# A Fourier transform and two MLPs: the feature transform folded into the first weights, the 64-point transform moved into the first block

## The reference

```
X = np.fft.fft(np.fft.fft(x, axis=1), axis=2).real
h = X @ w_in;   g = np.where(h > 0, h, np.exp(np.minimum(h, 0)) - 1);   x = g @ w_out
h = x @ w_in2;  g = np.maximum(h, 0) + alpha * np.minimum(h, 0);         out = g @ w_out2
```

## Time and profile before

| what | us |
|---|---|
| times of three runs | 1038.32, 1039.86, 1041.12 |
| median | 1039.86 |
| span of the profiled execution | 1040.5 |
| TensorE busy | 1018.8 (98% of the span) |
| ScalarE busy | 673.9 (65%) |
| VectorE busy | 652.1 (63%) |
| POOL busy | 112.6 (11%) |

### The profile page before, as it was taken

One profiled execution on the slowest core, in us unless ns is written; L12 is line 12 of the kernel. 1 busy time (PEld: TensorE's weight loads), 2 busy tenths in 40 slices (PEclk: granted clock), 3 DMA queues, 4 the chain that ended last, 5 costly groups with the idle time before them and its releaser, 6 DMA issues.

```text
span 1040.5 us, 13229 instructions
## 1 busy us (share of the span) xinstructions
PE 1018.8 (98%) x4858; PEld 861.7 (83%) x4858; DVE 652.1 (63%) x676; ACT 673.9 (65%) x769; POOL 112.6 (11%) x101
## 2 busy tenths in 40 slices
PE   6799899999999999999999999999999999999998
PEld 6799788888888888888888888888888888888886
DVE  4344888988889888888855544544545454544444
ACT  3343787888888878887866556556655656555553
POOL 3693121212120210000000000000000000000000
PEclk9899999999999999999999999999999999999999
DMA  8637300302102002011020010002002001000101
GB/s 226 164 125 267 106 21 11 111 10 67 54 20 101 10 0 91 0 41 41 1 77 0 1 63 18 0 0 81 0 0 81 0 0 43 34 1 1 41 1 42
DMA packets 17358, 50.64 MB, mean 49 GB/s; under 512 B 1520, under 2 KB 10032, under 8 KB 14640
## 3 DMA queue, kind: packets, MB, share of 16 engines
q1 hardware_dynamic: 14208, 40.70, 11.7%
q0 software_dynamic: 3120, 9.54, 3.1%
HBM read 29.92 MB, written 20.32 MB: 48 GB/s over the span
## 4 chain that ended last, share of the span: by engine, by line
PE 95%; DMA 2%; DVE 2%; ACT 1%; issue 0%; SPq 0%; DVEq 0%; ACTq 0%
PE ACC L447 16%; PE ACC L448 16%; PE ACC L452 16%; PE PQ L431 8%; PE PQ L430 8%; PE PQ L429 8%; PE PQ L323 2%; PE PQ L400 2%; PE PQ L401 2%; PE PQ L406 2%; PE PQ L402 2%; PE PQ L405 2%; PE PQ L407 2%; PE PQ L404 2%; DMA xr<-in_x 2%; PE PQ L352 1%
## 5 line engine op out<-in xcount | busy, mean ns | idle before, releaser
L447 PE MATMUL ACC<-Gh,W 128*128 128x512 f32 (+1 forms) x768 | 297.1, 387 | 1.8 <-DVE eo_st L705 1.0
L448 PE MATMUL ACC<-Gl,W 128*128 128x512 f32 (+1 forms) x768 | 296.2, 386 | 0.0
L743 DVE TENSOR_TENSOR Gl<-G,Gh 128x1024 fp32r<-128x1024 f32 (+1 forms) x96 | 115.4, 1203 | 212.5 <-ACT Gh L562 212.5
L452 PE MATMUL ACC<-Gh,W 128*128 128x512 f32 (+1 forms) x768 | 233.9, 386 | 0.0
L641 ACT ACTIVATE H<-PQ 128x1024 f32<-128x1024 f32 (+1 forms) x96 | 97.1, 1011 | 130.4 <-PE PQ L431 130.4
L447 PEld LDWEIGHTS ACC<-Gh,W 128*128 128x128 f32 x768 | 144.1, 188 | 34.6 <-issue 2.7
L448 PEld LDWEIGHTS ACC<-Gl,W 128*128 128x128 f32 x768 | 144.3, 188 | 28.2
L452 PEld LDWEIGHTS ACC<-Gh,W 128*128 128x128 f32 x768 | 143.4, 188 | 25.1
L562 ACT ACTIVATE Gh<-G 128x1024 fp32r<-128x1024 f32 (+1 forms) x96 | 100.1, 1042 | 74.1 <-PE ACC L452 70.4
L430 PE MATMUL PQ<-y_hl,W 128*128 (+2 forms) x384 | 148.0, 385 | 0.0
L431 PE MATMUL PQ<-y_hl,W 128*128 (+2 forms) x384 | 148.0, 385 | 0.0
(11 more groups left out here) (78 smaller groups left out, 1148.8 us busy)
## 6 DMA issues: line engine op xcount, KB each, us to landing
eo_scratch<-eo_st SPq DMA_DIRECT2D x12, 640.0 KB, 3.9
EO<-eo_scratch SPq DMA_DIRECT2D x6, 1280.0 KB, 7.9
xr<-in_x SPq DMA_DIRECT2D x16, 384.0 KB, 6.9
raw<-in_w POOLq DMA_DIRECT2D x24, 256.0 KB, 3.2
y_scratch<-y_st SPq DMA_DIRECT2D x5, 1024.0 KB, 4.8
y_in<-y_scratch SPq DMA_DIRECT2D x5, 1024.0 KB, 6.9
out_y<-y_st SPq DMA_DIRECT2D x5, 1024.0 KB, 4.8
stage<-in_w1a POOLq DMA_DIRECT2D x4, 256.0 KB, 5.5
```

Source lines behind the costliest of these rows:

```text
L447: mm(o, W[:, 0, sl], Gh[:, j, c:c + w], start=f == 0, stop=False)
L448: mm(o, W[:, 0, sl], Gl[:, j, c:c + w], start=False, stop=False)
L452: ins = mm(o, W[:, 1, sl], Gh[:, j, c:c + w], start=False, stop=f == NF - 1)
L743: tt(Gl[:, j, 0:n], G[:, j, 0:n], f32(Gh[:, j, 0:n]), ALU.subtract).then_inc(lo_ready, 1)
```

## The change

The d_model transform is linear, and so is the first MLP's up product. It is multiplied into w_in on the chip: eight pieces of two fp32 matmuls (fold_w1) between the chunks of stage one give W1, which ScalarE and VectorE split. The 64-point transform is done in fp32 with 128 columns a matmul, on T1 kept in fp32, and one tile at a time: tile 0 ahead of block 1, tile t + 1 at step 8 of tile t. Its output is E and O by itself, and goes to EO in SBUF without DRAM. The row for the Nyquist feature comes from three small matmuls, a diagonal matrix that VectorE makes and an fp32 matmul with ones (spread). Stage one's result is copied, not split: ScalarE the first half of each chunk, VectorE the second. The hardware loops are written out. The tile order ends with frequency 0. POOL splits W3 and W4 at one piece per step, from the last transform on.

```diff
-TILE_K2 = list(range(K2T, K2)) + list(range(K2T))
+TILE_K2 = list(range(K2T, K2)) + list(range(1, K2T)) + [0]
...
+W34_PACE = 1
...
+FLIP_AT = 8
...
+    T1 = at("T1", o2, [PT, C47, PT], fp32)
...
+    wn = at("wn", o4 + 16 * KB, [PT, 2, F], fp32)
+    mcw = at("mcw", o4 + 32 * KB, [PT, 2, 2, PT], fp32)
...
+    mcf = at("mcf", o6, [PT, 2 * PT + N1 + PT], fp32)
...
-            for u in range(NU):
-                if u:
-                    sp.wait_ge(eo_stored, 16 * u)
-                if u == NU - 1:
-                    sp.wait_ge(ym_ready, 1)
-                else:
-                    sp.wait_ge(eol_ready, u + 1)
-                j = u % 2
-                sp.dma_start(eo_dram[u // 2, :, :, j * SUB:(j + 1) * SUB], f32(eo_st[:, j, :, :])).then_inc(
-                    eo_stored if u < NU - 1 else y_stored, 16)
...
-                load_eo(t + 2, t % 2)
...
-            for k in range(8):
-                if k:
-                    gp.wait_ge(f1_done, 2 * k)
-                sl = slice(k % 4 * F // 4, (k % 4 + 1) * F // 4)
-                gp.dma_start(stage1[:, k // 4, sl], (w1a, w1b)[k // 4][:, sl]).then_inc(w_in[0], 16)
...
+            gp.dma_start(mcw[:, :, :, :], cw).then_inc(cw_in, 16)
+            for c in range(4):
+                sl = slice(c * 512, (c + 1) * 512)
+                gp.dma_start(wn[:, 0, sl], wa[:, sl]).then_inc(wn_in[c], 16)
+                gp.dma_start(wn[:, 1, sl], wb[:, sl]).then_inc(wn_in[c], 16)
+            gp.dma_start(mcf[:, :], cf).then_inc(cf_in, 16)
+            gp.dma_start(alpha_sb[:, :], alpha).then_inc(alpha_in, 16)
...
-            chain(gp.tensor_tensor(tmp, a, b, ALU.add))
-            split(W1[:, :, 0, :], W1[:, :, 1, :], by_f(tmp))
-            chain(gp.tensor_tensor(tmp, a, b, ALU.subtract))
-            split(W1[:, :, 2, :], W1[:, :, 3, :], by_f(tmp))
...
+            gp.wait_ge(w1l_ready, 8)
+            for p, part in ((0, 2), (32, 3), (64, 2)):
+                gp.dma_start(f32(W1e[p:p + 1, :]).rearrange("p (f c) -> p f c", f=NF), f32(W1[0:1, :, part, :])).then_inc(w1e_in, 16)
+            gp.wait_ge(w1e_in, 48)
+            gp.memset(f32(W1[0:1, :, 2:4, :]), 0.0).then_inc(w1_ready, 1)
...
                 if k == after_w2:
-                    gp.wait_ge(y_stored, 16)
+                    gp.wait_ge(f2_done, NT)
                 if k > after_w2:
-                    gp.wait_ge(down_done, W34_PACE * (k - after_w2))
-                loads[k % 2] += 16
-                gp.wait_ge(w_in[k % 2], loads[k % 2])
...
+            def fold_w1(i):
+                c, which = i // 2, i % 2
+                sl = slice(c * 512, (c + 1) * 512)
+                if which == 0:
+                    pe.wait_ge(wn_in[c], 32)
+                if i >= 4:
+                    pe.wait_ge(w1l_ready, i - 3)
+                o = ACC[:, i % 4, :]
+                mm(o, mcw[:, 0, which, :], wn[:, 0, sl], start=True, stop=False)
+                mm(o, mcw[:, 1, which, :], wn[:, 1, sl], start=False, stop=True).then_inc(w1_done, 1)
...
+            flip1(0)
+            flip1(1)
+            pe.wait_ge(cw_in, 16)
+            for c in range(2, NX):
+                if c - 2 < 8:
+                    fold_w1(c - 2)
...
+            def flip2(t):
+                if t == 0:
+                    pe.wait_ge(t1a_ready, NX)
+                    pe.wait_ge(t1b_ready, NX)
+                else:
+                    pe.wait_ge(comb_ready, NF * (t - 1) + FLIP_AT - 1)
...
+                for q in range(NQ):
+                    k2, b = TILE_K2[t * K2T + q // B], q % B
+                    o = PQ[:, 0, q * PT:(q + 1) * PT]
...
-                        mm(o, T1h[:, c, :], m64[:, cs, 0, :], start=n == 0, stop=False)
-                        mm(o, T1h[:, c, :], m64[:, cs, 1, :], start=False, stop=False)
-                        ins = mm(o, T1l[:, c, :], m64[:, cs, 0, :], start=False, stop=n == len(parts) - 1)
+                        ins = mm(o, T1[:, c, :], m64[cs], start=n == 0, stop=n == len(parts) - 1)
...
-            def final(u):
-                pe.wait_ge(uvl_ready, u + 1)
-                if u >= 2:
-                    pe.wait_ge(eol_ready, u - 1)
...
+            def spread(t):
+                pe.wait_ge(diag_ready, t + 1)
+                if t:
+                    pe.wait_ge(comb_ready, NF * (t - 1) + FLIP_AT)
+                mm(PQ[:, 1, 0:TW], ones, diag[t % 2][:, :], start=True, stop=True).then_inc(e_done, 1)
...
+                if t < LAST and f == FLIP_AT:
+                    pe.wait_ge(eol_ready, t + 2)
+                if t < LAST and f == FLIP_AT + 1:
+                    pe.wait_ge(el_ready, t + 2)
...
+            for s in range(3, S1):
+                t, f = s // NF, s % NF
+                if f == FLIP_AT and t < LAST:
+                    flip2(t + 1)
+                    spread(t + 1)
+                    down1(s - 3)
+                    up1(t, f)
+                else:
+                    up1(t, f)
+                    down1(s - 3)
...
+            def t1_copy(c):
+                src = PQ[:, c % 2, 0:TW].rearrange("p (s c) -> p c s", s=XH)[:, 0:C47, :]
+                act.wait_ge(f1_done, 2 * c + 1)
+                fn(T1[:, :, c * XD:c * XD + XH], src, ACT.Copy).then_inc(t1a_ready, 1)
...
+            def w1_hi(i):
+                c, which = i // 2, i % 2
+                act.wait_ge(w1_done, i + 1)
+                fn(W1[:, 4 * c:4 * c + 4, 2 * which, :], ACC[:, i % 4, :].rearrange("p (f c) -> p f c", f=4), ACT.Copy).then_inc(w1h_ready, 1)
...
+            def eo_hi(t):
+                act.wait_ge(f2_done, t + 1)
+                fn(eo(t, 0, 2).rearrange("p (e q k) -> p e q k", e=2, k=N1),
+                   PQ[:, 0, :].rearrange("p (q e k) -> p e q k", e=2, k=N1), ACT.Copy).then_inc(eoh_ready, 1)
+            def e_hi(t):
+                act.wait_ge(e_done, t + 1)
+                fn(eo(t, 4), PQ[:, 1, 0:TW], ACT.Copy).then_inc(eh_ready, 1)
...
+                flip_next = f == FLIP_AT - 1 and t < LAST
...
+                if flip_next:
+                    eo_hi(t + 1)
+                    e_hi(t + 1)
+                    copy_q(s + 1)
...
+            def t1_copy(c):
+                src = PQ[:, c % 2, TW:2 * TW].rearrange("p (s c) -> p c s", s=XH)[:, 0:C47, :]
+                dve.wait_ge(f1_done, 2 * c + 2)
+                nc.vector.tensor_copy(T1[:, :, c * XD + XH:(c + 1) * XD], src).then_inc(t1b_ready, 1)
...
+            def w1_lo(i):
...
+            def make_diag(t):
+                u = U128[:, NQ * t:NQ * (t + 1)].unsqueeze(2).to_broadcast([N1, NQ, N1])
+                i = eye.unsqueeze(1).to_broadcast([N1, NQ, N1])
+                tt(diag[t % 2][:, :].rearrange("p (q k) -> p q k", k=N1), u, i, ALU.mult).then_inc(diag_ready, 1)
...
+            def eo_lo(t):
+                dve.wait_ge(eoh_ready, t + 1)
+                tt(eo(t, 2, 2).rearrange("p (e q k) -> p e q k", e=2, k=N1),
+                   PQ[:, 0, :].rearrange("p (q e k) -> p e q k", e=2, k=N1),
+                   f32(eo(t, 0, 2)).rearrange("p (e q k) -> p e q k", e=2, k=N1), ALU.subtract).then_inc(eol_ready, 1)
+            def e_lo(t):
+                dve.wait_ge(eh_ready, t + 1)
+                em = eo(t, 4)[PT // 2:PT, :]
+                tt(em, PQ[PT // 2:PT, 1, 0:TW], f32(em), ALU.subtract).then_inc(el_ready, 1)
...
+                after_flip = f == FLIP_AT and t < LAST
...
+                if f == FLIP_AT - 3 and t < LAST:
+                    make_diag(t + 1)
+                if f == FLIP_AT - 1 and t < LAST:
+                    g_lo(s - 1, -1.0)
+                    elu(s)
+                    eo_lo(t + 1)
+                    e_lo(t + 1)
+                if t == LAST and f - 1 in SPLIT_AT:
```

More of the change, by code:

```diff
@@ L103, in program @@
-    W4 = at("W4", q + 76 * KB, [PT, 2, NF * D], f32r)
-    warm = at("warm", q + 108 * KB + 1536, [PT, 1], fp32)
+    T1 = at("T1", o2, [PT, C47, PT], fp32)
+    W4 = at("W4", o2, [PT, 2, NF * D], f32r)
+    W3h = at("W3h", o2 + 32 * KB, [PT, ND * F], f32r)
+    o3 = o2 + 48 * KB
+    EO = at("EO", o3, [PT, 2 * EOW], f32r)
+    diag = [at(f"diag{j}", o3 + 4 * (j * EOW + 4 * TW), [N1, TW], fp32) for j in range(2)]
+    y_in = at("y_in", o3, [PT, YW], fp32)
+    o4 = o3 + 20 * KB
+    H = at("H", o4, [PT, 2, 2 * TW], fp32)
@@ L106, in program @@
+    W3l = at("W3l", o5, [PT, ND * F], f32r)
+    o6 = o5 + 16 * KB
+    mcf = at("mcf", o6, [PT, 2 * PT + N1 + PT], fp32)
+    U128 = at("U128", o6 + 1792, [N1, B * K2], fp32)
+    warm = at("warm", o6 + 2048, [PT, 1], fp32)
+    m64 = [mcf[:, cs * PT:(cs + 1) * PT] for cs in range(2)]
+    m64x = [mcf[N1:PT, cs * PT:(cs + 1) * PT] for cs in range(2)]
+    eye = mcf[0:N1, 2 * PT:2 * PT + N1]
+    ones = mcf[0:N1, 2 * PT + N1:2 * PT + N1 + PT]
     with ExitStack() as ctx:
@@ L505, in _ @@
+            for f in range(3):
+                up2(0, f, TW)
+                down1(S1 - 3 + f)
+            for s in range(3, S1):
+                up2(s // NF, s % NF, width(s) - TW)
+                down2(S1 + s - 3)
```

(28 more changed lines are left out.)

716 lines of the change are left out of this document (243 added, 473 removed).

## The result

The changed kernel takes 1023.44 us (median of four runs, 1022.46 to 1024.11), the kernel before 1039.72 beside it (1038.32 to 1041.12). The ratio is 0.9843, with an interval from 0.9829 to 0.9857: 1.6% faster, 16.3 us. The forecast was 1013; the time lies inside the stated range, and outside the likeliest case's own range of 1008 to 1019. The profiled execution took 1023.8 us, 2.1 more than its span of 1021.7.

What follows compares the result with a forecast made beforehand. TensorE was taken as the bound: 68.0 us to the first down product, 923.9 for the rest as before and 22.2 for added transforms make 1014.1 of span; less 0.6, 1013.5, written 1013. Range 1004 to 1026.

Steps and rivals of the forecast that it cites:

- the likeliest case: Whole kernel: the forecast of 1013 us, with its own range of 1008 to 1019 us and a chance of 0.61.
- the 56.9 us: Between input stage and block 1: TensorE time of the removed transforms, 474 matmuls by 0.12 us.
- Wide fp32 matmuls: Folds and broadcasts: a 512-column fp32 matmul goes by columns, 0.91 us each; 14.5 us for the folds' 16.
- the cheap bound of 0.45: Folds and broadcasts: each record of a wide fp32 matmul costs no more than an f32r one, 0.453 us a matmul.
- the second rival: Folds and broadcasts: wide fp32 matmul is weight-bound; 7.2 and 2.3 us less, 1004 us; chance 0.1.
- The input stage: Start of kernel: x's chunk 1 lands at 9.1 us, then 23 items of 1.81 us; stage ends at 50.8 us.
- The third rival: Input stage starves, as all weights are ahead of x at once: 1019 to 1023 us; chance 0.08.
- the fourth rival: Written-out loops: straight-line code isn't fetched in time, slower than before, 1062 us in one case; chance 0.04.
- The transforms inside block 1: Five tiles: 78 products, 17.7 us, and five broadcasts, 4.5 us; 22.2 us on TensorE's path, no wait.
- Fill of block 1: Start of block 1: first up product at 59.0 us, first down product at 68.0 us, with 2.6 us idle.
- "Cost zero" for W3 and W4: Block 1: POOL's pieces, one per step, cost nothing, as VectorE has 0.56 us a step free.
- the span sum of 1014.1: Whole kernel: 68.0 + 923.9 + 22.2 us of span, against 1040.5 before.

Runs made afterwards that it cites:

- experiments 4 and 5: Changed kernel: 4 without the second matmul of each fold, 1018.02 us; 5 with the 64-point products of the five tiles inside block 1 done twice, 1041.45 us.
- experiment 7: Kernel before, with the low-order terms of its d_model stage left out (120 matmuls): 1037.39 us, ratio 0.9975 to the kernel before.
- experiment 2: Changed kernel with all 16 POOL pieces of W3 and W4 released four down products later: 1024.18 us, ratio 0.9831 to the kernel before.
- experiment 3: Changed kernel with 9 and 11 extra fp32 products in TensorE's two gaps before the first up and first down product: 1021.09 us.
- experiment 1: Changed kernel with W4 split from tile 3's transform on and W3 behind tile 5's, so POOL idles before the last tile: 1019.57 us.

## Why the prediction was right or wrong, point by point

**The mechanism was right for the changed kernel, and so were most terms.** TensorE is the bound there, and a microsecond of it is one of the span (experiments 4 and 5: 6.8 us removed gave 6.4 of span, 17.7 added gave 17.6). For the kernel before, the prediction's sentence that a microsecond taken out of the middle is one off the end is wrong between input stage and block 1: 14.4 us taken out there gave 2.8 (experiment 7). The sum didn't suffer from it, because the stores and loads went together with the matmuls, and because it goes by positions and not by the 56.9 us.

**Wide fp32 matmuls.** Right: 0.86 us against the 0.91 taken, and the cheap bound of 0.45 is excluded, the second rival with it. By the Trainium skill, TensorE: Matmul & The Clock Gate, on fast weight load, the wide form might have been cheap. The four passes of the Trainium skill, FP8 and Floating Point Precision (TensorE Precision Notes), are what the trace agrees with, 0.86 us being 3.8 f32r matmuls of that width.

**The input stage.** 50.19 us against 50.8, and part of that is luck. The prediction had TensorE wait 2.3 us for x's second chunk. In the changed kernel's profile it didn't: the first two chunks are one unbroken piece, but their 16 products took 5.61 us and not 3.6, as TensorE ran at half rate until 8.5 us (records 0.21 us apart and not 0.11), which the sum didn't have. With the 0.7 us for wn's first piece and folds of 0.86 us and not 0.91, the terms nearly cancel. The third rival didn't come here. A small form of it is in two of the nine profiles with the fold: in experiment 2's, x's second chunk was waited for 0.5 us, the half rate went on to about 14 us, and the stage ended at 52.44. One reading was off as well: between 30 and 40 us the kernel before waited 1.36 us for VectorE's T1l and only 0.35 for x.

**Code fetch.** 36 packets instead of 19, as foreseen, and no wait: the fourth rival didn't come.

**The transforms inside block 1.** No wait, as worked out. Their price was under-sized: the pair of steps around a transform grew by 4.85 us in four tiles and 4.40 in the last, 23.8 in all instead of 22.2. TensorE there, and the two VectorE splits:

```profile
91.41 3.73 PE L300 MATMUL PQ<-mcf,T 128*128 128x128 f32 x32
95.07 1.12 PE L308 MATMUL PQ<-diag,mcf 64*128 64x512 f32 x2
96.12 0.50 PE L379 MATMUL ACC<-Gh,W 128*128 128x512 f32 x1
...
98.97 0.39 PE L335 MATMUL PQ<-EO,W 128*128 128x512 f32 x1
```

```profile
96.26 1.22 DVE L582 TENSOR_TENSOR EO<-PQ,EO 128x1024 fp32r<-128x1024 f32 x1
97.51 0.69 DVE L589 TENSOR_TENSOR EO<-PQ,EO 64x512 fp32r<-64x512 f32 x1
```

The products themselves take 3.66 us (3.62 taken); the broadcast takes 1.05 from its start to the next down product's (0.91 taken), and the down product behind it 2.85 instead of 2.72. The low part of EO ends at 97.48, 1.5 us ahead of the up product that waits for it: the spare was 0.9 by the prediction.

**Fill of block 1: the failed step.** From the first up product to the first down product the prediction counted 9.0 us; it took 11.1. It had named the risk that the clock falls after an idle piece, allowed one microsecond in each of the two, and put none into the sum. The clock cost 0.9 us ahead of the first down product and 1.6 behind it (experiment 3). The rows of before had a price for it: the chunk at 43.92, behind an idle piece of 2.1 us, took 3.22 us for 16 records, where 64 took 7.41; so the clock was down there already, and not only at 48 us as the prediction has it. Another 0.8 us are VectorE's join and low part, 1.66 and 1.57 us instead of 1.22, with W2's pieces on POOL beside them. The prediction had called these pieces hidden, as they are ready in time; it put at nothing what they take from VectorE. Some 0.3 us are hand-offs. At full clock the first down product comes at 68.21, close to the predicted 68.0, but only because the first up product came 0.5 us early; the stretch between the two is 9.7 us there, and not 9.0.

**"Cost zero" for W3 and W4: the other failed step.** It said that VectorE's loss would fit in the 0.56 us that it has free per step. In steps 75 to 79 that was right. In the last tile it lost 1.1 us at once in a step, on the chain that a down product waits for; 3.2 us in all (experiment 1). The mean of a window gave room; the piece of POOL that starts just ahead of the join doesn't.

**The rest.** Against the span sum of 1014.1 the measured 1021.7 is 7.6 more: 1.7 ahead of the first down product, and 5.9 behind it, of which 1.6 are the cold down product, 1.6 the transforms, 3.2 the last tile, less 0.5 by which the steps right behind it and the first steps of a tile are shorter than in the kernel before. The remaining 2.3 us of the 9.9 between 1013.5 and 1023.44 are the step from span to time: the profiled execution of before had a span of 1040.5, while the spans of its runs beside the experiments had a median of 1038.7 and times some 1.8 us longer. The prediction took its offset of -0.6 from a span that was itself on the long side.

**Removed stages.** The 56.9 us were credited with the trip through DRAM counted as hidden. That was right for the kernel before, but only by a narrow margin (experiment 7), which the prediction didn't see, though the DMA engines' share in the window from 90 us was 0.70.

## What to carry to other kernels

When TensorE is the bound, price a moved transform by its columns and passes, and then look at every idle gap that the new order opens on TensorE: the gap costs its length and then, in most of the profiles here, again what the lower clock takes from the matmuls behind it; move independent matmuls into it, or spend extra ones. A share of free time in a window doesn't say that two engines can overlap there: where POOL and VectorE work at once, look at the length of single instructions in the steps in question, and at which of the two starts first. Work of POOL that is ready in time isn't free by that. And a transfer that costs nothing today may be the second bound just behind the first: thin the first one to find out.

## What the runs showed of the hardware that was not expected

- VectorE's join of 896 columns took 2.18 us instead of 1.08 when a POOL subtraction of 512 columns was under way at its start, and POOL's took 2.01 instead of 1.30. The Trainium skill, GPSIMD Engine Reference, Key points, lists contention of the SBUF interfaces that POOL shares with VectorE when a VectorE instruction has two SBUF inputs, as this join does. The trace agrees: the join ended 0.94 us behind POOL's instruction. With the join first, it kept its 1.22 us (1024 columns), and a POOL rounding that started 0.02 us behind it took 1.68 instead of 0.62.
- TensorE's granted clock went to its lower level after a gap of only 2.1 us (matmuls 0.43 us apart from 59.97 to 63.33 us) and again after one of 2.75 us (70.04 to 73.42), and stayed at the upper one when the gaps were filled. In two other executions it stayed at the upper one after idle pieces of 3.0 and 3.35 us.
- An fp32 matmul of 512 columns costs 0.86 us, 3.8 times a 512-column f32r one.
